# First two chunks of a recurrent attention: products issued beside the mask, with PSUM banks of their own

## What is computed

```
f = sigmoid(f_logit)
for t in range(S):
    state = f[t, :, None] * state + outer(k[t], v[t])
    y[t] = q[t] @ state
x  = rows of y, width 384
xn = x / sqrt(mean(x*x) + 1e-6) * rms_g
x2 = (silu(xn @ w_gate) * (xn @ w_val)) @ w_out        # inner width 1536
h  = x2 @ w_in                                         # inner width 2048
g  = h if h >= 1, 0 if h <= -1, else (h + 1)**2 / 4
out = g @ w_out2
```

## Time and profile before

| | |
|---|---|
| median of 3 runs | 931.78 us (931.78 to 931.91) |
| the profiled execution, its own time | 932.1 us |
| its span, first to last instruction | 930.3 us |
| granted clock of PE | 1.00 |
| instructions in the profile | 18649 |

### The profile page before, as it was taken

How to read it: one execution, slowest core, us unless ns; L and a number is a source line. 1 busy time by engine, 2 the same in 40 slices (tenths; PEclk the granted TensorE clock), 3 DMA queues, 4 the chain that set the end, 5 groups by cost and what they waited for, 6 DMA issues and landing times.

```text
span 930.3 us, 18649 instructions
## 1 busy us (share of the span) xinstructions
PE 921.4 (99%) x7498; PEld 784.6 (84%) x7498; DVE 555.1 (60%) x975; ACT 329.7 (35%) x563; POOL 15.6 (2%) x35
## 2 busy tenths in 40 slices
PE   7999999999999999999999999999999999999998
PEld 5999999998888888888888888888888888888886
DVE  8987658757656575575555555445445545454453
ACT  4653333332223232332233434243333433433333
POOL 1000000000000000000000000000000000000000
PEclk9999999999999999999999999999999999999999
DMA  9622533532422442243313100000000000000000
GB/s 316 238 70 71 160 91 100 178 97 86 141 79 66 137 129 72 81 123 101 102 51 99 38 1 0 1 34 0 28 6 0 34 0 0 34 0 0 35 1 35
DMA packets 52277, 65.90 MB, mean 71 GB/s; under 512 B 14576, under 2 KB 42992, under 8 KB 52208
## 3 DMA queue, kind: packets, MB, share of 16 engines
q1 hardware_dynamic: 52064, 64.75, 22.0%
q10 hardware_dynamic: 144, 0.13, 0.0%
HBM read 51.43 MB, written 13.43 MB: 70 GB/s over the span
## 4 chain that ended last, share of the span: by engine, by line
PE 97%; issue 2%; POOL 0%; ACT 0%; DVE 0%; POOLq 0%
PE gate_ps L630 16%; PE val_ps L630 16%; PE acc L708 14%; PE acc L652 11%; PE gate_ps L696 11%; PE val_ps L696 11%; PE acc L712 7%; PE acc L656 5%; PE pair_ps L470 2%; PE y_ps L493 2%; PE y_ps L532 2%; PE pair_ps L521 1%; PE acc L723 0%; PE pair_ps L453 0%; POOL columns L440 0%
## 5 line engine op out<-in xcount | busy, mean ns | idle before, releaser
L994 ACT ACTIVATE raw<-raw,columns 128x512 f32<-128x512 f32 x96 | 69.4, 723 | 155.2 <-DVE raw L1454 155.2
L708 PE MATMUL acc<-high,low 128*128 128x512 f32 x282 | 109.9, 390 | 0.0
L708 PE MATMUL acc<-high 128*128 128x512 f32 x282 | 109.8, 390 | 0.0
L652 PE MATMUL acc<-high 128*128 128x512 f32 (+2 forms) x252 | 90.1, 362 | 0.0
L652 PE MATMUL acc<-high,low 128*128 128x512 f32 (+2 forms) x252 | 89.4, 359 | 0.0
L1001 ACT ACTIVATE high<-qd 128x512 fp32r<-128x512 f32 x96 | 60.7, 632 | 73.3 <-DVE qd L1459 73.3
L712 PE MATMUL acc<-low,high 128*128 128x512 f32 x282 | 79.2, 389 | 0.0
L1454 DVE TENSOR_SCALAR raw<-val_ps 128x512 f32<-128x512 f32 x48 | 33.2, 691 | 76.5 <-PE val_ps L696 76.5
L1454 DVE TENSOR_SCALAR raw<-gate_ps 128x512 f32<-128x512 f32 x48 | 33.1, 689 | 61.9 <-PE gate_ps L696 61.6
L1391 DVE TENSOR_TENSOR low<-qd,high 128x512 fp32r<-128x512 f32 x96 | 65.7, 684 | 5.7 <-ACT high L1001 5.1
L630 PE MATMUL gate_ps<-high 128*128 128x512 f32 (+2 forms) x249 | 65.1, 369 | 0.1
(11 more groups left out here) (153 smaller groups left out, 1700.3 us busy)
## 6 DMA issues: line engine op xcount, KB each, us to landing
raw<-qkf_dram SPq DMA_DIRECT2D x22, 770.0 KB, 4.7
x_all<-wb_dram SPq DMA_DIRECT2D x12, 576.0 KB, 5.9
kd_turn_dram<-after SPq DMA_DIRECT2D x19, 256.0 KB, 2.9
kd<-kd_turn_dram SPq DMA_DIRECT2D x76, 64.0 KB, 2.6
v_sb<-v_dram SPq DMA_DIRECT2D x23, 192.0 KB, 2.6
v_early<-v_dram SPq DMA_DIRECT2D x23, 192.0 KB, 2.9
out_dram<-x_all SPq DMA_DIRECT2D x5, 768.0 KB, 3.8
x_turn_dram<-x_all SPq DMA_DIRECT2D x19, 192.0 KB, 1.9
```

Of the source, the lines that this page charges most:

```text
L652: pe.matmul(acc[:, m, 0:width(i)], wb_part(w, j, 2, m), h_hi[:, j % 2, 0:width(i)], start=(j == 0 and w is w_hi), stop=False)
L708: pe.matmul(acc[:, m, 0:N2], wc_part(w, j, 1, m), h2_hi[:, j % 2, :], start=(j == 0 and w is w_hi), stop=False)
L994: nc.scalar.activation(act2_buf[:, j % 2, :], act2_buf[:, j % 2, :], ACT.Square, bias=half_col[:, :], scale=0.5).then_inc(square_ready, 1)
```

## The change

For chunks 0 and 1 the scores go to two banks of `acc` (`first_scores`) in place of `pair_ps`. In `attend` of these chunks the update products come first, then the state products, then the wait for the masked scores, then the second outputs. The outputs of chunk 1 go to `gate_ps` (`second_y`) in place of `y_ps`, so its state products don't wait for `xs_ready` 1; their squares are written into `scores`. Chunk 0's x and both k are transposed into `val_ps`, and `turn_x(0)` follows `attend(1)`. The parts of chunk 1 go through the three banks of `acc`. One `keep_warm` of one product is taken out. On DVE `decay_q(1)` is ahead of `update_state(0)`, `mask_scores(1)` ahead of `normalise(0)`, `update_state(1)` ahead of `rest_x(0)`. `decay_after(2)` moves from the start into slot 2 of the first tile and `decay_k` of chunk 2 from slot 1 to slot 3; on ACT `sigmoid_f(2)` moves from the start to slot 0, and `square_sum(1)` ahead of `round_x(0)`. DVE gets one more memset of one column.

```diff
@@ -72,7 +72,7 @@
 STAGE, STAGES = 3, 5
 
 
-WARM_START, WARM_SCORES, WARM_LAST = 2, 1, 2
+WARM_START, WARM_LAST = 2, 2
 AHEAD = 3
 
 
@@ -160,8 +160,10 @@
         pair_ps = ctx.enter_context(nc.psum_tensor("pair_ps", [P, 2, 512], F32))
         tb, ta = pair_ps[:, 0, :], pair_ps[:, 1, :]
         score_ps = pair_ps[:, :, 0:2 * UP].rearrange("s r (a t) -> s r a t", a=NP // 2)
-        turned_x = gate_ps
-        turned_parts = val_ps, acc[:, 1, :], acc[:, 2, :]
+        turned_parts = [acc[:, k, :] for k in range(KM)]
+        second_y = gate_ps[:, 0:DM + 1]
+        first_scores = acc[:, 1:3, 0:2 * UP].rearrange("s r (a t) -> s r a t", a=NP // 2)
+        second_squares = scores[:, :, :, :].rearrange("p r h t -> p (r h t)")[:, 0:DM + 1]
         update_ps = pair_ps[:, :, 2 * UP:2 * UP + 2 * D]
 
 
@@ -455,6 +457,7 @@
 
                 def score(n, c):
 
+                    made = first_scores if isinstance(n, int) and n < FIRST else score_ps
                     for a in range(NP // 2):
                         for h in range(2):
                             keys = slice(h * HP, (h + 1) * HP)
@@ -462,7 +465,7 @@
                                 p = 2 * a + odd
                                 for r in range(2):
                                     rows = slice(r * HP, (r + 1) * HP)
-                                    to = score_ps[keys, r, a, :].rearrange("s (j t) -> s j t", t=HP)
+                                    to = made[keys, r, a, :].rearrange("s (j t) -> s j t", t=HP)
                                     if h == odd:
                                         to, q = to[:, 0:2 + odd:1 + odd, :], qd[rows, half(n, c), p, :]
                                     else:
@@ -482,21 +485,26 @@
                     pe.sem_inc(score_begun, 1)
                     score(n, c)
 
+                def outputs(n):
+                    return second_y[:, 0:DM].rearrange("t (r p e) -> t r p e", r=2, p=NP) if n == 1 else y_heads
+
                 def attend_state(n, c):
 
                     pe.wait_ge(wide_ready, n + 1)
-                    if n > 0:
+                    if n > 1:
                         pe.wait_ge(xs_ready, n)
                     for p in range(NP):
                         for s in range(C // QW):
                             q = slice(s * QW, (s + 1) * QW)
-                            pe.matmul(y_heads[q, :, p, :], qd[0:PR, half(n, c), p, q],
+                            pe.matmul(outputs(n)[q, :, p, :], qd[0:PR, half(n, c), p, q],
                                       wide[0:PR, p, :].rearrange("d (r e) -> d r e", r=2),
                                       start=(p == 0), stop=False, skip_group_check=True)
 
                 def attend(n, c, scores_next=False):
 
-                    pe.wait_ge(scores_ready, n + 1)
+                    early_chunk = isinstance(n, int) and n < FIRST
+                    if not early_chunk:
+                        pe.wait_ge(scores_ready, n + 1)
                     values, early = v_sb, v_early
                     if isinstance(n, int) and n == 1:
                         pe.wait_ge(v_second_loaded, 32)
@@ -515,20 +523,24 @@
                     if scores_next:
                         pe.wait_ge(qd_ready, n + 2)
                         pe.wait_ge(kd_ready, n + 2)
-                    attend_state(n, c)
+                    if not early_chunk:
+                        attend_state(n, c)
                     for p in range(NP):
                         for b in range(NB):
                             mm = pe.matmul(update_ps[b * BS:(b + 1) * BS, p // 2, p % 2 * D:(p % 2 + 1) * D],
                                            kdT[:, b, p, :], values[:, b // 2, p, :], start=True, stop=True)
                     mm.then_inc(update_made, 1)
+                    if early_chunk:
+                        attend_state(n, c)
+                        pe.wait_ge(scores_ready, n + 1)
                     for r in range(2):
                         for a in range(NP // 2):
                             for s, odd in ((0, None), (2, 0), (1, None), (3, 0), (2, 1), (3, 1)):
                                 q = slice(s * QW, (s + 1) * QW)
                                 if odd is None:
-                                    y, t, given = y_heads[q, r, 2 * a:2 * a + 2, :], s * QW, early[:, r, a, :]
+                                    y, t, given = outputs(n)[q, r, 2 * a:2 * a + 2, :], s * QW, early[:, r, a, :]
                                 else:
-                                    y, t, given = y_heads[q, r, 2 * a + odd, :], s * QW + odd * HP, values[:, r, 2 * a + odd, :]
+                                    y, t, given = outputs(n)[q, r, 2 * a + odd, :], s * QW + odd * HP, values[:, r, 2 * a + odd, :]
                                 mm = pe.matmul(y, scores[:, r, a, t:t + QW], given,
                                                start=False, stop=True, skip_group_check=True)
                     mm.then_inc(y_made, 1)
@@ -583,14 +595,13 @@
 
                     pe.wait_ge(f_loaded, 16)
                     keep_warm(WARM_START)
-                    turn_kd(0, acc[:, 1, :])
+                    turn_kd(0, val_ps)
                     score_alone(0, 0)
-                    keep_warm(WARM_SCORES)
                     attend(0, 0)
-                    turn_kd(1, acc[:, 1, :])
+                    turn_kd(1, val_ps)
                     score_alone(1, 1)
-                    turn_x(0, turned_x)
                     attend(1, 1)
+                    turn_x(0, val_ps)
                     keep_warm(WARM_LAST)
                     for k, bank in enumerate(turned_parts):
                         if k < KM - 1:
@@ -789,6 +800,11 @@
 
                 def square_sum(n):
                     act.wait_ge(y_made, n + 1)
+                    if isinstance(n, int) and n == 1:
+                        act.wait_ge(xs_ready, 1)
+                        nc.scalar.activation(second_squares, second_y, ACT.Square, scale=DM ** -0.5, accum_out=ssq[:, :])\
+                            .then_inc(ssq_ready, 1)
+                        return
                     if isinstance(n, int) and n < CARRIED:
                         if n > 0:
                             act.wait_ge(xT_made, n)
@@ -817,7 +833,9 @@
                     for c in range(SIZES[1]):
                         n = FIRST + c
                         o = slot - WINDOW * c
-                        if o == 0 and c == 1:
+                        if o == 0 and c == 0:
+                            sigmoid_f(n)
+                        elif o == 0 and c == 1:
                             sigmoid_f(n, raw_second)
                         elif o == 0 and c == 2:
                             sigmoid_f(n)
@@ -1027,14 +1045,13 @@
                 nc.scalar.activation(unused[:, :], half_col[:, :], ACT.Sigmoid)
                 sigmoid_f(0)
                 sigmoid_f(1, raw_second)
-                copy_kdT(0, acc[:, 1, :])
+                copy_kdT(0, val_ps)
                 square_sum(0)
-                copy_kdT(1, acc[:, 1, :])
+                copy_kdT(1, val_ps)
                 widen(1)
                 split_wb(0)
-                round_x(0, 0, turned_x)
-                sigmoid_f(2)
                 square_sum(1)
+                round_x(0, 0, val_ps)
                 split_wb(1)
                 round_parts()
                 sigmoid_gate(0, 0)
@@ -1129,7 +1146,7 @@
                     dve.wait_ge(scores_made, n + 1)
                     if not isinstance(n, int) or n > 0:
                         dve.wait_ge(y_made, n)
-                    nc.vector.tensor_tensor(scores[:, :, :, :], score_ps,
+                    nc.vector.tensor_tensor(scores[:, :, :, :], first_scores if isinstance(n, int) and n < FIRST else score_ps,
                                             causal[:, :].unsqueeze(1).unsqueeze(1)
                                             .to_broadcast([P, 2, NP // 2, UP]), ALU.mult).then_inc(scores_ready, 1)
 
@@ -1148,9 +1165,10 @@
 
                 def normalise_parts():
                     dve.wait_ge(rstd_ready, 2)
+                    dve.wait_ge(xT_made, 1)
                     for k in range(KM):
                         columns = slice(k * P, (k + 1) * P)
-                        nc.vector.scalar_tensor_tensor(out=xs[:, columns], in0=y_ps[:, columns], scalar=rstd[:, :],
+                        nc.vector.scalar_tensor_tensor(out=xs[:, columns], in0=second_y[:, columns], scalar=rstd[:, :],
                                                        in1=g_rows[:, columns], op0=ALU.mult, op1=ALU.mult)\
                             .then_inc(xs_part_ready if k < KM - 1 else xs_ready, 1)
 
@@ -1192,11 +1210,9 @@
                         n = FIRST + c
                         inputs = raw_second if c == 1 else raw
                         o = slot - WINDOW * c
-                        if o == 1 and c == 0:
-                            decay_k(n, c)
-                        elif o == 1:
```

(11 more changed lines are left out.)

## The result

The changed kernel takes 936.30 us (median of 14 runs, 933.81 to 938.34), the kernel before 932.12 in its 14 (931.67 to 936.50). The ratio is 1.0036, with a 95% interval of 1.0026 to 1.0047: slower, by some 3.4 us by the ratio; the two medians lie 4.2 us apart. The profiled execution took 935.95 us, with a span of 934.2.

The account below looks back on a forecast made before the run. PE was taken as the bound, busy 921.4 of 930.3 us, with DVE also full in the first MLP tile. Terms 0 + 0.1 + 2.11 - 0.02 gave +2.2 us, so 934.0 from 931.78; 8-in-10 range 932.6 to 935.3.

Parts of the forecast that it names:

- First chunk: Chunk 0 in the start: update and state products start near 9.95, and y_made(1) comes 1.0 us earlier.
- Second chunk, the landing: Chunk 1 in the start: attend(1) waits for v_second to land at 16.2, so y_made(2) stays at 18.1: 0 us.
- (a): Rival for chunk 1: the landing of v_second does not bind; -0.84 at the first gate, +1.3 in all, 933.1; chance 0.17.
- (b): Rival for the first tile: DVE's lateness does not reach PE, so not slower, 931.9 us; chance 0.06.
- (d): Rival for chunk 0: updates can't run beside the mask, y_made(1) stays at 12.9; still 934.0, chance within the main case.
- To the first gate: From y_made(2) to the first gate product: turn_x(0) ahead of the warming makes the transposes later, +0.1 us.
- The tile: First tile of the MLP: moved sigmoid and scan make DVE 2.11 us later; PE stalls about 1.7, score(2) 2.1 later.
- The sum: Whole kernel: the terms add to +2.2 us, which from the median of 931.78 gives 934.0.
- rival (c): PE's clock falls between 12.5 and 16.2 us, attend(1) at half rate: some +2 on top, 936 us; chance 0.07.
- The sign that I had named: In chunk 1, products of attend(1) longer than 2.5 us would show that PE's clock had fallen.

Follow-up runs that it names:

- e8: The kernel before with only v_second issued early; attend(1) starts 0.06 us after the mask ends at 15.73; no total time is given.
- e5: The changed kernel with sigmoid_f(2), decay_after(2), decay_k moved back, one warming product after turn_kd(1), v_second issued early: 931.93 us, ratio 0.9992.
- e7: The changed kernel with only v_second issued earlier: median 933.02 us at full clock, clock low in 3 of 12 runs.
- e2: The kernel before with only the hand-over: sigmoid_f(2) to slot 0, decay_after(2) to slot 2, decay_k of chunk 2 to slot 3: 933.85 us, ratio 1.0020.
- e3: The changed kernel with two warming products, one after the transposes of k of chunk 1, one between score(1) and attend(1): median 933.92 us.
- e9: The changed kernel with the removed warming product put back between score(0) and attend(0); clock low in 6 of 12 runs; no median is given.
- e6: The kernel before with only decay_after(2) in slot 2 and decay_k of chunk 2 in slot 3, the sigmoid left in the start: 934.19 us, one run.
- e4: The changed kernel with the edits of both e1 and e3: 932.27 us, ratio 1.0004.
- e10: The kernel of e5 with the two loads of v of chunk 2 issued behind y_made 2 instead of y_made 1: 931.76 us, ratio 0.9994.
- e1: The changed kernel with sigmoid_f(2) and decay_after(2) back in the start and decay_k of chunk 2 back in slot 1: median 934.38 us.
- e12: The changed kernel with one warming product, after the transposes of k of chunk 1: median 934.22 us, clock low in 5 of 12 runs.

## Why the prediction was wrong, point by point

The direction was right, and so was the largest term; the size was missed, since the measured median lies 1.0 us above the range.

- **First chunk: right.** L530 at 9.81 (said: 9.95), and transposes of k one microsecond earlier.
- **Second chunk, the landing: right.** qd, score and mask came within 0.05 us of the forecast. The row of attend(1) names the transfer, and e8 shows what is there without it. The landing was at 15.7 in this run, not 16.2. Behind it stood a wait that I had not seen, with no semaphore (by my reading, for PE's next piece of code): with v early it, and not the mask, held the state products (e5, e7).
- **The other rivals.** (a), that the landing does not bind, falls with e8. (b), that DVE's lateness does not reach PE, falls with e2. (d), that the updates can't run beside the mask, falls with the rows at 9.81 and 10.17, as the mask runs from 10.00.
- **To the first gate: close at full clock.** From the start of attend(1) to the first gate product e3 takes 4.65 us and e9 4.66 (16.17 to 20.82, 16.33 to 20.99); before it was 4.78 (16.23 to 21.01). I said 0.1 more than before, and it is 0.1 less.
- **The tile: right.** Said +2.11 for rest_h(0,0), measured +2.06; said a stall of 1.7, measured 1.61; said score(2) 2.1 later against the gate, measured 2.03, and 2.05 from the moves alone. The split by cause holds too (e6).
- **The sum: right for the runs it describes, in part by luck.** 934.0 against 934.04 in the five runs at full clock. But the 931.78 that I started from is 0.3 below the 932.12 of the 14 runs of before, so the step at full clock is nearer 1.9 us than my 2.2; e3's trace gives 1.85, -0.19 at the gate and +2.04 from there to score(2) (32.35).
- **The clock: wrong.** The step that failed is rival (c), with its chance of 0.07, and the sentence behind it that after each short gap the products run at full pace. The trace had two gaps, 0.6 us each, ahead of 14.1 and 16.2; the change makes them 1.44 and 0.84 us (the latter 1.64 in e9, where v_second landed later) and leaves only score(1) between. From gaps that did no harm I took it that longer ones would not. The clock fell in 9 of 14 runs. One execution also hid that the kernel before is near this edge: its clock is low in 17 of the 97 runs taken beside the experiments, and those take 934.0 us or more. The sign that I had named came: attend(1) took 3.7 us (15.71 to 19.38), where 2.5 was the bound. The size was short as well: I said some 2 us, and the median of the nine runs is 2.8 above that of the five. My own terms, 1.9 for attend(1) and 1.8 for four warming records at 0.94 in place of 0.50, add up to 3.7 less the 0.19 to spare, and not to 2. In the profiled run only the first came: from attend(1) to the gate product it takes 6.45 us, 1.8 more than e3 and e9, and the warming runs at full rate (1.88 us from 19.70). As v_second landed some 0.5 earlier than in before, the gate product is only 1.15 later.
- **Left open.** The profiled run loses a further 0.7 us between 166 and 179 us, at the gap at 178.01 above and one of 0.23 us ahead of 179.04. Ahead of them ACT waits 2.3 us for a load of raw inputs (1.3 before), and scan, rest_h and PE follow. e9's profile, with the same code order there, has no such loss, so I take it for the loads of that run, but nothing was tried on it.

The page that I cited, of the Trainium skill (TensorE: Matmul & The Clock Gate, "The HAM clock gate"), spoke for rival (c) in its rule that too little activity brings the throttled clock back. The windows of the changed kernel agree, with 0.50 from 16.0 to 19.0; I gave its rule too little weight against a trace that showed nothing of the kind.

## What to carry to other kernels

Ask of every step that is moved out of a prologue what the engine does where it lands: a scan of 1.2 us and a sigmoid of 0.6, free in a wait, cost 2.0 in a stage in which two engines were full. An overlap that lets PE finish early makes its next wait longer, and the clock then has to be counted in runs, not read in one trace: fill the waits, or keep the filler that is there. And before reordering products around a wait, look for the load that ends just as they begin, since it will be the next wait.

## What the runs showed of the hardware that was not expected

- The clock is lost by chance at the same code: full in all 46 runs of e3, e4, e5 and e10, low in 9 of 14 in the changed kernel, 5 of 6 in e1, 3, 6 and 5 of 12 in e7, e9 and e12, and in 17 of 97 runs of the kernel before. Of these 97 it is 5 of 30, 4 of 29, 2 of 21 and 6 of 17 in the four sets, each on another chip, so only runs of one set should be compared.
- PE can stop for 0.8 to 1.9 us in the middle of a group of products with no semaphore behind it, at a fixed place of its program (after 31 products, or 29 with two more pairs ahead), while the DMA engines are full (a share of 0.95 to 1.15 from 15.0 to 16.8 us in e1, e5 and e7, 0.86 in e10). It did not show in the profiles in which PE started these products at 15.7 us or later (e3, e4, e9, e12).
- The same transfer of 192 KB, issued at 9.4 to 9.5 us, landed after 6.0 to 7.7 us in the traces of different kernels. In the changed order this moves the first gate product by as much: it is at 20.38 in e12, where attend(1) starts at 15.72, and at 20.99 in e9, where it starts at 16.33.
